# Index columns of gathers and scatters set by VectorE from PSUM tables, one packed schedule word for GpSimd, four splits placed after the second routing

## The chip, the cores and the metric

One NeuronCore of a Trainium2 chip runs the whole program. The metric is the device time of one launch in microseconds (us); the median of several runs is compared.

## The reference

The input is q, k and v (batch 4, 8 heads, 576 rows, head width 64). Attention runs within chunks of 64 rows; its output is a matrix x of 2304 tokens by 512. Two mixtures of 8 experts follow, each with top-1 routing, hidden width 1024 and a relu. The second keeps at most 576 tokens for each expert.

```python
def mixture(x, w_gate, w1, w2):              # twice; the first also scales by an output gate
    logits = x @ w_gate                      # 2304 x 8
    e = argmax(logits); gate = softmax(logits)[e]
    for each expert: out[rows of e] = gate * (relu(x[rows] @ w1[e]) @ w2[e])
```

Everything is float32, and so is the output (2304 x 512).

## The kernel before

The engines run separate programs that wait on semaphores. Four stages follow one another: attention with the first router's logits, the first routing, the expert tiles of mixture m=0, then the second routing and the expert tiles of mixture m=1.

**Routing (L701 to L792, VectorE).** It takes the argmax of the logits, ranks the tokens within their expert by matmuls, gives each expert whole tiles of 128 slots, and makes tables with one column for each tile (NTAB columns, 128 partitions): `gather_at` (the token row that each slot reads), `scatter_at` (the row that it writes), `gates`, `owner` (the tile's expert). Every instruction in `link(...)` is waited for before the next is issued. From `owner_f` it also works out a schedule for GpSimd (called POOL in the profile): `pieces[m][g]` and `pieces[m][g+1]` say from which to which weight piece GpSimd has to work in step g, and `middles[m][g]` where the scatter and the gather stand between them. The last instruction (L791) raises `routed`, for which TensorE's first transposes of gathered rows (L993), VectorE's `x_split` and GpSimd's third gather wait. `index_ready`, after L763, releases the first gather earlier.

**Weights.** A product is made of three matmuls (L998 to L1000) of a high and a low part, so that each weight piece (128 x 1024, 512 KB, 8 for each expert, 128 in all) goes through three steps: SyncE loads it into a ring of four slots, ScalarE copies it rounded into `wh` (L607; for an expert two further on, only when the last tile of the expert that holds the space has been multiplied), and GpSimd subtracts into `wl` (L423, called a split here). A split frees the ring slot. The pieces have one order through both mixtures. The first 12 are split during attention. In m=0 the schedule covers pieces 12 to 76. Pieces 76 to 80 (the second half of expert 1 of m=1) are split in the second routing, between its first and second gather (L497 to L499), and m=1's schedule starts at 80.

**A tile's way.** There are 20 tiles in each mixture. GpSimd gathers 128 rows into `xg` (indirect DMA, L514, or L488 for the first three). TensorE transposes them (L993), VectorE splits them into high and low parts (L812, L814), TensorE makes the first product (L998 to L1000), VectorE the relu (L804), TensorE transposes (L1020), VectorE splits (L821, L827), TensorE makes the second product, VectorE scales it into `y` (L842), and GpSimd scatters `y` (L528). In m=0 TensorE and VectorE also make the next router's logits of `y` (L1039, L835, L1045, L846), which the scatter writes along. TensorE's step g is: transposes of tile g, first product of tile g+1, transposes of the rows of tile g+2, second product of tile g. There is one `xg`, one `y`, one `gidx` and one `sidx`: L842 of tile j waits until the scatter of tile j-1 has landed (`y_out`), and the gather of tile g waits for the transposes of tile g-1 (`xT_done`).

**GpSimd's step g (L532 to L541)**, in program order: three loads of schedule values into registers (`due`, L434 to L436), the splits from lo to middle (at most 4), the scatter of tile g-1, the gather of tile g+3 (not in the last two steps), the splits from middle to hi. Before the scatter it copies a column of `scatter_at` into `sidx` (L522) and waits for its own copy, and before the gather a column of `gather_at` into `gidx` (L511), since the indirect DMA takes its indices from a fixed address.

Of the kernel before, what the change touches and what calls it, by code (L numbers as in the profile page):

```python
# [13 lines left out]
P = 128  # L14
# [9 lines left out]
def build(nc, q, k, v, wg1, wog1, w1a, w2a, wg2, w1b, w2b, cap, out):  # L24
# [31 lines left out]
    with ctx:  # L56
# [61 lines left out]
        scatter_at = [sb(f"scatter_at{m}", [P, NTAB], I32) for m in range(2)]  # L118
# [3 lines left out]
        pieces = [sb(f"pieces{m}", [P, NTAB], I32) for m in range(2)]  # L122

        middles = [sb(f"middles{m}", [P, NTAB], I32) for m in range(2)]
# [57 lines left out]
        ps_rank, ps_slot, ps_gate = b6, b7, b45  # L182

# [69 lines left out]
        si_here = [sem(f"si_here{m}") for m in range(2)]  # L253
# [141 lines left out]
        def _(pool):  # L395
# [35 lines left out]
            def due(m, g):  # L431


                lo = pool.value_load(at(pieces[m], g)[0:1, :], min_val=PX, max_val=2 * E * PX)  # L434
                hi = pool.value_load(at(pieces[m], g + 1)[0:1, :], min_val=PX, max_val=2 * E * PX)
                middle = pool.value_load(at(middles[m], g)[0:1, :], min_val=PX, max_val=2 * E * PX)  # L436
                return lo, middle, hi
# [14 lines left out]
            for m in range(2):  # L452
# [44 lines left out]
                if m == 1:  # L497
                    for i in range((E + 1) * PX + PW, (E + 2) * PX):
                        low_parts(i, i % RING)  # L499
                    pool.wait_ge(s_zero, 16 * NT)  # L500
# [5 lines left out]
                def gather(g):  # L506

                    if reached(g, 1):
                        pool.wait_ge(g_in[m], g * 16)
                        pool.wait_ge(xT_done[m], g)  # L510
                    nc.gpsimd.tensor_copy(gidx[:, :], at(gather_at[m], g)).then_inc(gi_here[m], 1)  # L511
                    pool.wait_ge(gi_here[m], g - 2)
                    stand_alone(pool)
                    nc.gpsimd.indirect_dma_start(xg[:, 0:src.shape[1]], None, src,  # L514
                                                 bass.IndirectOffsetOnAxis(ap=gidx[:, 0:1], axis=0),
                                                 bounds_check=N - 1, oob_is_err=False).then_inc(g_in[m], 16)

                def scatter(g):

                    if reached(g, 1):  # L520
                        pool.wait_ge(y_out[m], g * 16)
                    nc.gpsimd.tensor_copy(sidx[:, :], at(scatter_at[m], g)).then_inc(si_here[m], 1)  # L522
                    pool.wait_ge(si_here[m], g + 1)
# [111 lines left out]
        def _(dve):  # L635
# [65 lines left out]
            for m in range(2):  # L701
# [64 lines left out]
                for k in range(2):  # L766
# [16 lines left out]
                done = FIRST if m == 0 else (E + 2) * PX  # L783
                link(nc.vector.tensor_scalar_add(pace[:, 0:MT], pace[:, 0:MT], float(m * E * PX)))
                link(nc.vector.tensor_scalar(pieces[m][:, 1:MT + 1], pace[:, 0:MT], float(done), float(2 * E * PX),
                                             ALU.max, ALU.min))
                link(nc.vector.memset(pieces[m][:, 0:1], done))
                link(nc.vector.scalar_tensor_tensor(out=middles[m][:, 0:MT], in0=pieces[m][:, 0:MT], scalar=float(PW),
                                                    in1=pieces[m][:, 1:MT + 1], op0=ALU.add, op1=ALU.min))
                link(nc.vector.tensor_scalar(padding[:, :], slot_n[:, :], 0.0, float(SKIP), ALU.is_equal, ALU.mult))  # L790
                nc.vector.scalar_tensor_tensor(out=scatter_at[m][:, :], in0=padding[:, :], scalar=-1.0,  # L791
# [7 lines left out]
                def relu(j, half):  # L799
# [4 lines left out]
                    nc.vector.tensor_scalar_max(h[:, cols], ps_h[:, cols], 0.0).then_inc((h0_here, h1_here)[half][m], 1)  # L804

# [31 lines left out]
                def scaled(j):  # L837

                    dve.wait_ge(y_done[m], j + 1)
                    if reached(j, 1):  # L840
                        dve.wait_ge(y_out[m], j * 16)
                    nc.vector.tensor_scalar(y[:, 0:D], ps_y, at(gates[m], j), None, ALU.mult).then_inc(y_here[m], 1)  # L842
# [5 lines left out]
                def step(g, head=False, tail=False):  # L848
# [18 lines left out]
                    if not tail:  # L867
                        relu(g + 1, 1)
                        x_split(g + 2)
# [232 lines left out]
```

## Time and profile before

| | |
|---|---|
| three runs | 753.7, 753.04, 751.76 us (median 753.04) |
| the profiled execution | 754.11 us |
| its span in the trace | 752.4 us |
| TensorE busy | 642.0 us, 85% |
| VectorE busy | 356.8 us, 47% |
| ScalarE busy | 180.3 us, 24% |
| GpSimd busy | 419.8 us, 56% |
| TensorE's mean granted clock | 0.929 |

All times in the rows are from the start of the span. Attention ends near 108, the first tile of m=0 starts at 124, the second routing is from 433 to 459, and the rest is m=1. Busy shares are means over these stages. The splits alone (L423) are 302 us of GpSimd's time. A row of the timeline is: start, duration, engine, line, operation, output and inputs, and in brackets the engine's idle time before it with what ended it.

### The profile page before, as it was taken

How to read it: one execution, taken by the hardware profiler on the slowest of the kernel's cores; microseconds unless marked ns; L12 is line 12 of the kernel's file. 1: busy time of each engine (PE TensorE's matmuls, PEld its weight loads, DVE VectorE, ACT ScalarE, POOL GpSimd, SP SyncE). 2: the span in 40 equal slices, each digit the busy share in tenths (PEclk: the TensorE clock that was granted, in tenths of full speed). 3: DMA queues.
4: the chain of work that ended last, by engine and by line, in shares of the span. 5: the costliest groups of instructions: out<-in, count | busy, mean ns of one | idle time of the engine just before them, and what ended most of it. 6: DMA issues, size and time to landing. Idle time of an engine off the chain costs nothing.

```text
span 752.4 us, 15054 instructions
## 1 busy us (share of the span) xinstructions
PE 642.0 (85%) x4310; PEld 529.1 (70%) x4311; DVE 356.8 (47%) x652; ACT 180.3 (24%) x223; POOL 419.8 (56%) x351
## 2 busy tenths in 40 slices
PE   4898855999999999999987534999999999998653
PEld 3787844788887888877876423788888878886542
DVE  3887745454354354354334084545454364433240
ACT  2577631002420112422322200022023200243200
POOL 1046442256685657779778342116657763579760
PEclk9999985999999999999998655999999999999796
DMA  9999993043444425445554313114325532355500
GB/s 198 233 297 283 271 337 125 29 140 137 157 156 152 154 79 174 175 154 186 178 176 155 110 37 104 44 34 153 126 87 177 182 126 84 112 174 195 191 32 21
DMA packets 79690, 111.64 MB, mean 148 GB/s; under 512 B 28249, under 2 KB 46681, under 8 KB 79664
## 3 DMA queue, kind: packets, MB, share of 16 engines
q1 hardware_dynamic: 67616, 86.00, 37.0%
q0 software_dynamic: 8000, 25.17, 9.9%
q10 hardware_dynamic: 4048, 0.12, 0.3%
q8 instruction: 17, 0.28, 0.2%
q14 instruction: 9, 0.07, 0.0%
HBM read 92.48 MB, written 20.00 MB: 150 GB/s over the span
## 4 chain that ended last, share of the span: by engine, by line
PE 50%; POOL 14%; issue 12%; DVE 10%; POOLq 5%; DMA 5%; ACT 1%; ACTq 1%; DVEq 0%; SPq 0%
PE b L998 12%; PE b L999 12%; POOL wl L423 12%; PE b L1000 12%; PE b L925 2%; PE b L1020 2%; PE b L993 2%; PE b L903 2%; DVE owner L773 1%; DVE kT L665 1%; POOLq L423 1%; PE b L1045 1%; DVE xrow L676 1%; DMA x<-y,sidx 1%; PE b L913 1%
## 5 line engine op out<-in xcount | busy, mean ns | idle before, releaser
L423 POOL TENSOR_TENSOR wl<-ring,wh (+1 forms) x128 | 302.0, 2386 | 43.0 <-issue 21.3
L607 ACT CAST wh<-ring 128x1024 f32 (+1 forms) x112 | 112.8, 1047 | 479.2 <-PE b L1000 387.3
L998 PE MATMUL b<-wh,xTh 128*128 x320 | 135.0, 422 | 5.7 <-DVE xTl L814 3.7
L998 PE MATMUL b<-wh,hTh 128*128 x320 | 132.5, 414 | 7.5 <-DVE hTl L827 7.5
L842 DVE TENSOR_SCALAR y<-b,gates 128x512 f32<-128x512 f32 x40 | 30.0, 751 | 227.0 <-PE b L1000 103.2
L999 PE MATMUL b<-wh,xTl 128*128 x320 | 129.0, 403 | 0.0
L999 PE MATMUL b<-wh,hTl 128*128 x320 | 128.9, 403 | 0.0
L1000 PE MATMUL b<-wl,xTh 128*128 x320 | 128.0, 400 | 0.0
L1000 PE MATMUL b<-wl,hTh 128*128 x320 | 127.9, 400 | 0.0
L804 DVE TENSOR_SCALAR h<-b 128x512 f32<-128x512 f32 x80 | 54.8, 689 | 78.3 <-PE b L1000 78.1
L998 PEld LDWEIGHTS b<-wh,hTh 128*128 128x128 f32 x320 | 61.8, 193 | 21.3 <-issue 7.7
L998 PEld LDWEIGHTS b<-wh,xTh 128*128 128x128 f32 x320 | 61.6, 193 | 19.1 <-issue 7.2
L1000 PEld LDWEIGHTS b<-wl,hTh 128*128 128x128 f32 x320 | 61.3, 192 | 15.1
L1000 PEld LDWEIGHTS b<-wl,xTh 128*128 128x128 f32 x320 | 61.3, 192 | 14.8
L999 PEld LDWEIGHTS b<-wh,hTl 128*128 128x128 f32 x320 | 61.8, 193 | 12.8
L999 PEld LDWEIGHTS b<-wh,xTl 128*128 128x128 f32 x320 | 61.8, 193 | 11.4
L514 POOL DMA_INDIRECT xg<-x,gidx x36 | 37.8, 1049 | 31.4 <-POOL gidx L511 30.5
L827 DVE TENSOR_TENSOR hTl<-b,hTh 128x512 fp32r<-128x512 f32 x80 | 52.7, 680 | 0.0
L821 DVE CAST hTh<-b 128x512 fp32r<-128x512 f32 x80 | 51.1, 681 | 0.0
L993 PE MATMUL b<-ident,xg 128*128 128x128 f32 x168 | 26.8, 284 | 25.2 <-DMA xg<-x,gidx 12.2
L427 POOL DMA_DIRECT2D x<-xrow x18 | 10.2, 566 | 63.3 <-DVE xrow L676 63.3
L993 PEld LDWEIGHTS b<-ident,xg 128*128 128x128 f32 x168 | 21.5, 147 | 32.3 <-DMA xg<-x,gidx 13.5
(142 smaller groups left out, 663.1 us busy)
## 6 DMA issues: line engine op xcount, KB each, us to landing
ring<-in_moe_w SPq DMA_DIRECT2D x128, 512.0 KB, 3.2
vin<-in_v SPq DMA_DIRECT2D x72, 64.0 KB, 4.9
x<-xrow POOLq DMA_DIRECT2D x18, 256.0 KB, 6.1
out<-zeros SPq DMA_DIRECT2D x18, 256.0 KB, 3.8
qin<-in_q SPq DMA_DIRECT2D x6, 512.0 KB, 7.5
kin<-in_k SPq DMA_DIRECT2D x6, 512.0 KB, 6.9
qin<-in_q SPq DMA_DIRECT2D x2, 384.0 KB, 5.6
kin<-in_k SPq DMA_DIRECT2D x2, 384.0 KB, 5.9
```

What stands on the lines that cost most here:

```text
L423: nc.gpsimd.tensor_tensor(low, src, high.bitcast(F32), ALU.subtract).then_inc(wl_here, 1)
L514: nc.gpsimd.indirect_dma_start(xg[:, 0:src.shape[1]], None, src, bass.IndirectOffsetOnAxis(ap=gidx[:, 0:1], axis=0), bounds_check=N - 1, o ...
L607: nc.scalar.copy(dst, ring[:, i % RING]).then_inc(wh_here, 1)
L804: nc.vector.tensor_scalar_max(h[:, cols], ps_h[:, cols], 0.0).then_inc((h0_here, h1_here)[half][m], 1)
L821: nc.vector.tensor_copy(hTh[:, chunks, :], ps_hT[:, half * BANK:(half + 1) * BANK].rearrange("p (c t) -> p c t", t=P)).then_inc((hTh0_here ...
L827: nc.vector.tensor_tensor(hTl[:, chunks, :], ps_hT[:, half * BANK:(half + 1) * BANK].rearrange("p (c t) -> p c t", t=P), hTh[:, chunks, :] ...
L842: nc.vector.tensor_scalar(y[:, 0:D], ps_y, at(gates[m], j), None, ALU.mult).then_inc(y_here[m], 1)
L903: last = nc.tensor.transpose(ps_aT[:, c * P:(c + 1) * P], xrow[:, (t - 1) % XS, c].rearrange("p e d -> p (e d)"), ident[:, :])
L993: last = nc.tensor.transpose(ps_xT[:, c * P:(c + 1) * P], xg[:, c * P:(c + 1) * P], ident[:, :])
L998: nc.tensor.matmul(dst, high, weights(wh, *wt), start=start, stop=False)
L999: nc.tensor.matmul(dst, low, weights(wh, *wt), start=False, stop=False)
L1000: return nc.tensor.matmul(dst, high, weights(wl, *wt), start=False, stop=stop)
```

## The change

- `due` loads one word, `schedule[m][g]`, which is lo + 256 middle + 65536 hi, and takes it apart in registers. VectorE makes the word in the routing with two more linked instructions. `pieces` and `middles` become float tables that both mixtures share.
- VectorE writes the two index tables into PSUM (`ps_gather`, `ps_scatter`, both in the bank b7, behind the columns that the routing's matmuls use there): one more linked instruction for `ps_gather`, while `scatter_at` becomes `ps_scatter`. `gather_at` stays in SBUF for the first three gathers.
- The copies into `gidx` and `sidx` move from GpSimd to VectorE: `next_rows(g + 3)` in VectorE's step g, after the relu of tile g+1 and before `x_split(g + 2)`, and the `sidx` copy in `scaled(j)`, after its waits and before L842. GpSimd's waits on `g_in`, `xT_done`, `y_out` and `si_here` ahead of these copies go with them. It now waits for `gi_here`, raised by VectorE, and for `y_here`.
- The four splits L497 to L499 leave the second routing. m=1's schedule starts at piece 76, so they come in its steps.

```diff
--- before.py
+++ after.py
@@ -115,13 +115,13 @@
 
         gates = [sb(f"gates{m}", [P, NTAB]) for m in range(2)]
         gather_at = [sb(f"gather_at{m}", [P, NTAB], I32) for m in range(2)]
-        scatter_at = [sb(f"scatter_at{m}", [P, NTAB], I32) for m in range(2)]
         ends = [sb(f"ends{m}", [P, E + 1], I32) for m in range(2)]
         owner = [sb(f"owner{m}", [P, NTAB], I32) for m in range(2)]
 
-        pieces = [sb(f"pieces{m}", [P, NTAB], I32) for m in range(2)]
-
-        middles = [sb(f"middles{m}", [P, NTAB], I32) for m in range(2)]
+        pieces = sb("pieces", [P, NTAB])
+
+        middles = sb("middles", [P, NTAB])
+        schedule = [sb(f"schedule{m}", [P, NTAB], I32) for m in range(2)]
 
         ring = sb("ring", [P, RING, PIECE])
 
@@ -180,6 +180,7 @@
         ps_pT, ps_aT = b6, b7
         ps_h, ps_hT, ps_y, ps_yT, ps_xT = b01, b23, b45[:, 0:BANK], b45[:, BANK:2 * BANK], b6
         ps_rank, ps_slot, ps_gate = b6, b7, b45
+        ps_gather, ps_scatter = b7[:, 2 * P:2 * P + NTAB], b7[:, 3 * P:3 * P + NTAB]
 
         s_const = sem("s_const")
         s_tables = sem("s_tables")
@@ -250,7 +251,6 @@
         yT_here = sem("yT_here")
         yl_done = sem("yl_done")
         yl_here = sem("yl_here")
-        si_here = [sem(f"si_here{m}") for m in range(2)]
         y_out = [sem(f"y_out{m}") for m in range(2)]
 
         w1_dram = [w.rearrange("e (c p) f -> e p c f", p=P) for w in (w1a, w1b)]
@@ -431,9 +431,8 @@
             def due(m, g):
 
 
-                lo = pool.value_load(at(pieces[m], g)[0:1, :], min_val=PX, max_val=2 * E * PX)
-                hi = pool.value_load(at(pieces[m], g + 1)[0:1, :], min_val=PX, max_val=2 * E * PX)
-                middle = pool.value_load(at(middles[m], g)[0:1, :], min_val=PX, max_val=2 * E * PX)
+                cuts = pool.value_load(at(schedule[m], g)[0:1, :], min_val=0, max_val=2 ** 24 - 1)
+                lo, middle, hi = pool.snap(cuts % 256), pool.snap(cuts // 256 % 256), pool.snap(cuts // 65536)
                 return lo, middle, hi
 
             def split(lo, hi):
@@ -495,8 +494,6 @@
                 pool.wait_ge(index_ready, m + 1)
                 gather_first(0)
                 if m == 1:
-                    for i in range((E + 1) * PX + PW, (E + 2) * PX):
-                        low_parts(i, i % RING)
                     pool.wait_ge(s_zero, 16 * NT)
                 gather_first(1)
                 pool.wait_ge(routed, m + 1)
@@ -505,10 +502,6 @@
 
                 def gather(g):
 
-                    if reached(g, 1):
-                        pool.wait_ge(g_in[m], g * 16)
-                        pool.wait_ge(xT_done[m], g)
-                    nc.gpsimd.tensor_copy(gidx[:, :], at(gather_at[m], g)).then_inc(gi_here[m], 1)
                     pool.wait_ge(gi_here[m], g - 2)
                     stand_alone(pool)
                     nc.gpsimd.indirect_dma_start(xg[:, 0:src.shape[1]], None, src,
@@ -517,10 +510,6 @@
 
                 def scatter(g):
 
-                    if reached(g, 1):
-                        pool.wait_ge(y_out[m], g * 16)
-                    nc.gpsimd.tensor_copy(sidx[:, :], at(scatter_at[m], g)).then_inc(si_here[m], 1)
-                    pool.wait_ge(si_here[m], g + 1)
                     pool.wait_ge(y_here[m], g + 1)
                     if m == 0:
                         pool.wait_ge(yl_here, g + 1)
@@ -780,15 +769,20 @@
                 link(nc.vector.tensor_scalar(near[:, 0:MT], near[:, 0:MT], float(PW), float(PX + PW), ALU.mult, ALU.add))
                 link(nc.vector.scalar_tensor_tensor(out=pace[:, 0:MT], in0=owner_f[:, 0:MT], scalar=float(PX),
                                                     in1=near[:, 0:MT], op0=ALU.mult, op1=ALU.add))
-                done = FIRST if m == 0 else (E + 2) * PX
+                done = FIRST if m == 0 else (E + 1) * PX + PW
                 link(nc.vector.tensor_scalar_add(pace[:, 0:MT], pace[:, 0:MT], float(m * E * PX)))
-                link(nc.vector.tensor_scalar(pieces[m][:, 1:MT + 1], pace[:, 0:MT], float(done), float(2 * E * PX),
+                link(nc.vector.tensor_scalar(pieces[:, 1:MT + 1], pace[:, 0:MT], float(done), float(2 * E * PX),
                                              ALU.max, ALU.min))
-                link(nc.vector.memset(pieces[m][:, 0:1], done))
-                link(nc.vector.scalar_tensor_tensor(out=middles[m][:, 0:MT], in0=pieces[m][:, 0:MT], scalar=float(PW),
-                                                    in1=pieces[m][:, 1:MT + 1], op0=ALU.add, op1=ALU.min))
+                link(nc.vector.memset(pieces[:, 0:1], float(done)))
+                link(nc.vector.scalar_tensor_tensor(out=middles[:, 0:MT], in0=pieces[:, 0:MT], scalar=float(PW),
+                                                    in1=pieces[:, 1:MT + 1], op0=ALU.add, op1=ALU.min))
+                link(nc.vector.scalar_tensor_tensor(out=middles[:, 0:MT], in0=pieces[:, 1:MT + 1], scalar=256.0,
+                                                    in1=middles[:, 0:MT], op0=ALU.mult, op1=ALU.add))
+                link(nc.vector.scalar_tensor_tensor(out=schedule[m][:, 0:MT], in0=middles[:, 0:MT], scalar=256.0,
+                                                    in1=pieces[:, 0:MT], op0=ALU.mult, op1=ALU.add))
                 link(nc.vector.tensor_scalar(padding[:, :], slot_n[:, :], 0.0, float(SKIP), ALU.is_equal, ALU.mult))
-                nc.vector.scalar_tensor_tensor(out=scatter_at[m][:, :], in0=padding[:, :], scalar=-1.0,
+                link(nc.vector.tensor_scalar(ps_gather, slot_n[:, :], -1.0, 0.0, ALU.add, ALU.max))
+                nc.vector.scalar_tensor_tensor(out=ps_scatter, in0=padding[:, :], scalar=-1.0,
                                                in1=slot_n[:, :], op0=ALU.add, op1=ALU.add).then_inc(routed, 1)
 
                 def gates_copy():
@@ -802,6 +796,11 @@
                         dve.wait_ge((hT0_done, hT1_done)[half][m], j)
                     cols = slice(half * BANK, (half + 1) * BANK)
                     nc.vector.tensor_scalar_max(h[:, cols], ps_h[:, cols], 0.0).then_inc((h0_here, h1_here)[half][m], 1)
+
+                def next_rows(g):
+
+                    dve.wait_ge(xT_done[m], g)
+                    nc.vector.tensor_copy(gidx[:, :], at(ps_gather, g)).then_inc(gi_here[m], 1)
 
                 def x_split(j):
 
@@ -839,6 +838,7 @@
                     dve.wait_ge(y_done[m], j + 1)
                     if reached(j, 1):
                         dve.wait_ge(y_out[m], j * 16)
+                    nc.vector.tensor_copy(sidx[:, :], at(ps_scatter, j))
                     nc.vector.tensor_scalar(y[:, 0:D], ps_y, at(gates[m], j), None, ALU.mult).then_inc(y_here[m], 1)
 
                 def logits_copy(j):
@@ -866,6 +866,7 @@
                         logits_copy(g - 1)
                     if not tail:
                         relu(g + 1, 1)
+                        next_rows(g + 3)
                         x_split(g + 2)
                     scaled(g)
                     if m == 0 and tail:
```

## Rows read from the trace of the kernel before

**Rows 1.** Waits of all engines: waiter, waited for, us in total, times, longest

```profile
DVE y L842 <- DMA out<-y,sidx: 63.9, 7, 17.4
```

**Rows 2.** Timeline, second routing (start us, duration us, work)

```profile
445.69 10.02 DVE L773 TENSOR_SCALAR owner<-owner_f 128x28 int32<-128x28 f32 x1
446.42 9.24 POOL L423 TENSOR_TENSOR wl<-ring,wh 128x1024 fp32r<-128x1024 f32 x4
...
459.29 1.11 PE L993 MATMUL b<-ident,xg 128*128 128x128 f32 x4 [11.34 <-DVE scatter_at L791]
```

**Rows 3.** Timeline, first routing, the same three places

```profile
120.30 0.18 DVE L773 TENSOR_SCALAR owner<-owner_f 128x28 int32<-128x28 f32 x1
...
123.17 0.19 DVE L791 SCALAR_TENSOR_TENSOR scatter_at<-padding,slot_n 128x28 int32<-128x28 f32 x1
...
124.27 1.11 PE L993 MATMUL b<-ident,xg 128*128 128x128 f32 x4 [1.70 <-DMA xg<-x,gather_at]
```

**Rows 4.** Timeline of POOL alone, one step of m=0

```profile
330.27 0.18 POOL L522 COPY sidx<-scatter_at 128x1 int32 x1
331.38 1.02 POOL L528 DMA_INDIRECT x<-y,sidx  x1 [0.93 <-POOL sidx L522]
332.39 0.20 POOL L511 COPY gidx<-gather_at 128x1 int32 x1
333.46 1.05 POOL L514 DMA_INDIRECT xg<-x,gidx  x1 [0.86 <-POOL gidx L511]
336.10 9.46 POOL L423 TENSOR_TENSOR wl<-ring,wh  x4 [1.59 <-ACT wh L607]
```

**Rows 5.** Line 434, one of the three loads: ns min/median/max

```profile
L434 POOLq TENSOR_LOAD <-pieces x40: 285/295/420, 136.8 to 727.6; - x40
```

**Rows 6.** Chain of work from 202 to 206: start, us, what

```profile
202.93 0.53 issue
```

**Rows 7.** Timeline of PE, m=0: transposes L1020 of tiles 0, 12, 13, 19

```profile
136.03 1.17 PE L1020 MATMUL b<-ident,h 128*128 128x128 f32 x8
...
303.81 1.04 PE L1020 MATMUL b<-ident,h 128*128 128x128 f32 x8
...
317.65 1.03 PE L1020 MATMUL b<-ident,h 128*128 128x128 f32 x8
...
406.46 1.03 PE L1020 MATMUL b<-ident,h 128*128 128x128 f32 x8
```

**Rows 8.** Timeline of DVE, m=0: L842 of tiles 18 and 19

```profile
409.31 0.75 DVE L842 TENSOR_SCALAR y<-b,gates 128x512 f32<-128x512 f32 x1 [6.68 <-DMA x<-y,sidx]
...
422.88 0.75 DVE L842 TENSOR_SCALAR y<-b,gates 128x512 f32<-128x512 f32 x1 [8.29 <-PE b L1000]
```

**Rows 9.** Stretch in m=0's last product: us, busy times, then PEclk, DMA share, GB/s

```profile
416.00:418.00 2.00, 2.00 (x6) 1.52 (x5) 0.00 (x0) 0.00 (x0) 2.00 (x1) 0.50 0.69 195
```

**Rows 10.** Timeline of PE, m=1: gathered tiles 12 and 19, transposes of tiles 13, 14

```profile
605.54 0.66 PE L993 MATMUL b<-ident,xg 128*128 128x128 f32 x4 [1.66 <-DMA xg<-x,gidx]
...
636.68 1.03 PE L1020 MATMUL b<-ident,h 128*128 128x128 f32 x8
...
649.20 1.03 PE L1020 MATMUL b<-ident,h 128*128 128x128 f32 x8
...
702.77 1.11 PE L993 MATMUL b<-ident,xg 128*128 128x128 f32 x4 [9.40 <-DMA xg<-x,gidx]
```

**Rows 11.** Timeline of POOL, m=1: splits of steps 15 and 16, scatter of 17

```profile
663.50 9.48 POOL L423 TENSOR_TENSOR wl<-ring,wh  x4 [1.99 <-ACT wh L607]
...
677.25 18.82 POOL L423 TENSOR_TENSOR wl<-ring,wh  x8
...
727.68 1.03 POOL L528 DMA_INDIRECT out<-y,sidx  x1 [0.94 <-POOL sidx L522]
```

**Rows 12.** Timeline of DVE, m=1: L842 of the last tile

```profile
741.30 0.75 DVE L842 TENSOR_SCALAR y<-b,gates 128x512 f32<-128x512 f32 x1 [7.57 <-PE b L1000]
```

**Rows 13.** Line 846, a small copy from PSUM: ns min/median/max

```profile
L846 DVE COPY y<-b x20: 166/166/167, 156.3 to 426.2; 128x8 f32<-128x8 f32 x20
```

## The prediction

> **What bounds the kernel now.** I read the waits first, then the timeline in three places. Busy shares name no bound: TensorE is busy for 85% of the span and GpSimd for 56%, but each is late in other stretches. Among the waits, VectorE's L842 (y) stands waiting for landed scatters of m=1, 63.9 us in 7 waits [rows 1]. A scatter is late only when GpSimd comes late to it. So the questions are where GpSimd's step is longer than TensorE's, and what else holds the path.
>
> Second routing: L773, a 128x28 instruction, takes 10.02 us [rows 2]; the same instruction in the first routing takes 0.18 [rows 3]. It ends at 455.71, and the four splits of GpSimd beside it end at 455.66 [rows 2]. The first routing has no splits beside it. TensorE then waits for `routed` until 459.29 [rows 2], so all of it is on the path.
>
> m=0: TensorE's tile takes 13.84 us when nothing is late (303.81 to 317.65) [rows 7]. GpSimd's step with four splits takes 15.24: in rows 4 the copy 0.18 and its wait 0.93, the scatter 1.02, the copy 0.20 and its wait 0.86, the gather 1.05, a gap of 1.59, and four splits of 9.41 in all. GpSimd is the bound wherever such steps follow one another. From tile 12 to 19 TensorE needs 102.65 us [rows 7], where seven tiles of 13.84 are 96.9: 5.8 us lost. From tile 0 to 12 it needs 167.8 against 166.1: 1.7 lost [rows 7]. At the end y of tile 18 waits for a scatter until 409.31, and y of tile 19 comes at 422.88 [rows 8], 16.4 us after tile 19's transposes; TensorE makes that last product at the granted clock of 0.50 (1.2 of 2.4 GHz) [rows 9].
>
> m=1: TensorE's tile takes 12.52 [rows 10]. It is stopped once for 1.66 by a late gather and once for 9.40 [rows 10], and at the end y of tile 18 is late again behind the scatter of tile 17 at 727.68 [rows 11].
>
> **The change part by part.**
>
> *Splits out of the second routing.* Without them L773 should take the 0.18 of the first routing and end at 445.87. From its end to the end of L791 the first routing takes 123.36 - 120.48 = 2.88 [rows 3]. Three linked instructions are new (two to pack the word, one for `ps_gather`), each of about 0.22 with its link, as L773 to L791 go (13 links in 2.88): 0.66 in all. L791 ends at 449.4, and TensorE starts 0.7 later (459.29 against L791's end), at 450.1. The other bound is the gather: in the first routing TensorE starts on the landed gather 3.97 after L773's start [rows 3], which gives 449.7 here, so it is covered. Gain 459.29 - 450.1 = 9.2. In the first routing the same three instructions cost 0.66, of which the gather's landing, by which TensorE waits there [rows 3], hides a part; bounds 0 and 0.66, I take 0.4.
>
> The trace shows one VectorE instruction held through four splits [rows 2]. The Trainium skill ("SBUF — State Buffer", "Who interferes with whom") says that a `tensor_scalar` with both operands in SBUF can take the port pair that VectorE shares with GpSimd, and that the second to come fully blocks; by that rule the stall goes with the splits, as the rows say.
>
> *Where the four splits land.* m=1's schedule now gives pieces 76 to 80 to step 1, ahead of the scatter of tile 0 and the gather of tile 4. They cost 9.4 there [rows 4]. TensorE makes expert 0's first tiles then, the scatter has to land only by the next y, a tile (12.5) after the last, and the gather waits for TensorE's transposes anyway. The splits run from about 482 to 492 in old times, the scatter lands some 3 us later, and the next y comes at 497.5. Cost 0, with 2.5 us to spare. SyncE's loads for expert 2 come later by as much and still ahead of ScalarE's need. If that cover were gone, it would cost up to 9.4.
>
> *Copies moved off GpSimd.* Each step loses 1.11 (330.27 to 331.38) and 1.07 (332.39 to 333.46) [rows 4]. That counts the wait: 0.53 of it is the sequencer preparing the indirect DMA after the copy [rows 6], which can now run ahead under the splits, since its semaphores stand long before. Of the gap of 1.59, two loads go, each 0.29 [rows 5] with about 0.3 of register work behind it; the divisions add something that no row shows, a few register operations. Bounds for the gap: 0 (all hidden) and 1.6 (the divisions eat the gain); I take 0.65, so 0.95 less. A step with four splits comes to 15.24 - 2.18 - 0.95 = 12.1, below both 13.84 and 12.52.
>
> VectorE gains two copies of 128x1 out of PSUM in a step. The nearest row is L846, also out of PSUM, at 0.166 [rows 13]. The `gidx` copy waits for the same transposes as the split of x behind it; what is queued behind is x_split, which TensorE needs a second product (about 6 us) later. The `sidx` copy delays y by 0.19; behind it stand the splits of the hidden tile, with over 4 us to spare, and in m=0 the transposes L1039, with 0.9. Both hidden, except once at each mixture's end: 0.4 in all. The gather now waits for VectorE in place of TensorE, 0.2 to 0.3 later, for rows needed a tile later: 0.
>
> *What that gives in m=0.* With steps of 12.1 every scatter lands within 0.3 of the moment that y wants, which the 0.9 covers, so both losses go: 1.7 + 5.8 = 7.5. At the end TensorE no longer stands still for 2.7 us before tile 18's logits, and its clock should stay up. Then y of tile 19 follows the transposes by 11.1 (0.6 + 0.9 to y of tile 18, 3.6 to its logits' end, 5.6 to 6 for the product) instead of 16.4: gain 5.3. With the clock down, as now, it is 2.5. I take 5.
>
> *What it gives in m=1.* The wait of 1.66 [rows 10] goes, since the gather before it leaves 5 us earlier: 1.7 to 1.9, I take 1.9. Steps 15 to 18 start from a split at 663.50 that ScalarE and TensorE set [rows 11] and stay there. Four splits end at 672.9; scatter and gather end at 675.1 in place of 677.2; eight splits in a row [rows 11] end at 693.9; scatter 694.0, gather 695.0 in place of 699.3, landed at 698.4. TensorE waits for it 5.2 instead of 9.4 [rows 10], and the second product of tile 17 starts at 700.2 (hidden splits behind y at 697.3) instead of 703.9. Then four splits from 696.8 to 706.2, scatter, gather to 708.3, and splits of the last four pieces from 709.0 (ScalarE can round them only after tile 17's product at 706.9) to 718.4. The scatter of tile 17 goes at 718.45 instead of 727.68 [rows 11], lands at 721.5, and y of the last tile follows by the same path as now, so 741.30 [rows 12] becomes 732.3. Gain 9.0, with 2 more if the clock stays up in the last product.
>
> *Sum.* 9.2 - 0.4 + 7.5 + 5 + 1.9 + 9.0 - 0.4 = 31.8. The span of 752.4 becomes 720.6 and the profiled run of 754.11 becomes 722.3. The median of the runs is 1.07 below that run, so I predict 753.04 - 31.8 = 721.2.
>
> **The rivals.**
>
> *The DMA can't be prepared ahead.* The gap between copy and DMA might be the DMA's own and be paid after any instruction. For: each indirect DMA of rows 4 shows it, and a scatter that waits for y shows 0.9 too. Against: the 0.53 stands behind the copy's semaphore [rows 6], and GpSimd's sequencer reads on while splits run. The copies then save only 0.2 each and the step is 13.9 long. m=0 still gets 7.1 + 4, m=1's end only 3.0 (steps 15 to 18: seven copies of 0.2 and two gaps of 0.8). Sum 9.2 - 0.4 + 7.1 + 4 + 1.9 + 3.0 - 0.6 = 24.2: 728.8. The Trainium skill ("Advanced Engine Details and Errata", "Sequencer Loop") has engine instructions queued while the sequencer reads on, which would speak for my forecast; no row shows a DMA queued so.
>
> *The copies are held by splits (slower).* If a 128x1 copy with integer output is held through a run of splits as L773 was (9.84 longer) [rows 2, 3], y waits on VectorE until the run ends. There are 29 runs of four splits behind the routings. With 4 us to spare in m=1 and 0.9 in m=0, a y that falls at a run's start would cost 5 to 8 us, perhaps 12 times: some 75. Then 753 - 22 + 75 = 806. It decides from 31.8 / 29 = 1.1 us of TensorE's time for each run. Against: L842 and L846 read PSUM under splits and are never stretched (0.166 to 0.167) [rows 13]; for: neither writes integers.
>
> *The packed word doesn't pay.* If the divisions take 1 us, the gap stays 1.6 and the step is 13.1, still below 13.84 but above 12.52. Only m=1's end notices: 2 us less, 723.
>
> **How the numbers follow.** Forecast with its variants of gap and clock 0.77, the unprepared DMA 0.15, held copies 0.05, no net change through a cover I misjudged 0.03. The range: below, 2.2 for the last product's clock, 1 for gaps hidden and 1 for the run: 717. Above, the second case and 2 for spread: 731. A difference of over 0.3% is what a measurement of this kernel can tell from none: faster 0.93, same 0.02, slower 0.05.
>
> **What would show it.** L773 near 0.18 in both routings, and TensorE's first transposes of m=1 about 4.4 us after it. GpSimd's step with four splits at 12.1 wherever it isn't waiting, with the scatter 0.1 behind the last split (0.9 would be the first rival). TensorE 13.84 a tile through all of m=0, and one wait of some 5 us for a gather in m=1. `sidx` and `gidx` copies near 0.16; any of several us is the slower case. I am wrong if splits in step 1 delay the first tiles, or if VectorE's copies show up ahead of TensorE's waits.

## The result and the profile after

The changed kernel takes 732.89 us (median of 4 runs, 731.08 to 733.94) against 753.37 (4 runs), a ratio of 0.972 with a 95% interval of 0.969 to 0.976. Timed a second time on another occasion it took 730.84 us (ratio 0.966, 0.964 to 0.968). I had forecast 721.2, with 717 to 731 as the range. The sign and most of the mechanisms were right; the gain was 20 to 25 us instead of 32.

The stages, read off the timelines of two profiled executions of each kernel. A stage begins and ends at the start of the instruction named.

| stage, us | before | after | forecast gain | gain |
|---|---|---|---|---|
| start to GpSimd's first copy of the gates in the first routing | 117.45, 121.23 | 120.41, 118.22 | 0 | none clear |
| to the first transposes of rows, m=0 | 6.82, 6.83 | 7.47, 7.48 | -0.4 | -0.65 |
| to the hidden transposes of tile 0 | 11.76, 11.75 | 11.71, 11.39 | 0 | 0.2 |
| to those of tile 19 | 270.43, 270.56 | 265.84, 265.56 | 7.5 | 4.8 |
| to the last y of m=0 | 16.42, 16.20 | 14.93, 14.81 | 4.8 | 1.4 |
| to the same copy of the gates, second routing | 19.97, 19.99 | 20.04, 20.10 | 0 | -0.1 |
| to the first transposes of rows, m=1 | 16.44, 16.44 | 7.28, 7.28 | 9.2 | 9.2 |
| to the hidden transposes of tile 0 | 11.54, 11.64 | 10.64, 10.60 | 0 | 1.0 |
| to those of tile 17 | 215.91, 216.06 | 214.00, 214.01 | 1.9 | 2.0 |
| to those of tile 18 | 23.87, 23.76 | 23.53, 23.50 | 3.8 | 0.3 |
| to those of tile 19 | 14.31, 14.44 | 12.52, 12.51 | 1.4 | 1.9 |
| to the last y, m=1 | 16.38, 16.30 | 12.63, 12.63 | 3.6 | 3.7 |
| to the end | 11.10, 11.10 | 11.10, 11.11 | 0 | 0 |

The two profiled executions of before took 754.11 and 758.01 us. Three rows hold the shortfall: m=0's tiles, m=0's end, and tile 17 to 18 of m=1. One row gave 1.0 that I hadn't forecast.

The second routing after the change, from the timeline of all engines (it answers rows 2):

```profile
442.81 1.13 POOL L487 DMA_INDIRECT xg<-x,gather_at  x1 [1.19 <-DVE gather_at L752]
...
443.24 0.18 DVE L762 TENSOR_SCALAR owner<-owner_f 128x28 int32<-128x28 f32 x1
...
446.77 0.20 DVE L785 SCALAR_TENSOR_TENSOR b<-padding,slot_n 128x28 f32<-128x28 f32 x1
447.68 1.11 PE L994 MATMUL b<-ident,xg 128*128 128x128 f32 x4 [2.19 <-DVE b L785]
```

L762 is the old L773. It takes 0.18, and TensorE starts 4.44 after it, still released by VectorE and not by the gather, as the 4.4 of the forecast had it.

GpSimd's steps in m=0, from its own timeline (they answer rows 4):

```profile
347.08 1.02 POOL L517 DMA_INDIRECT x<-y,sidx  x1
348.41 1.03 POOL L507 DMA_INDIRECT xg<-x,gidx  x1 [0.30 <-issue]
349.46 9.42 POOL L423 TENSOR_TENSOR wl<-ring,wh  x4
359.04 1.02 POOL L517 DMA_INDIRECT x<-y,sidx  x1 [0.17 <-DVE gidx L803]
360.37 1.02 POOL L507 DMA_INDIRECT xg<-x,gidx  x1 [0.31 <-issue]
361.42 9.44 POOL L423 TENSOR_TENSOR wl<-ring,wh  x4
371.44 1.02 POOL L517 DMA_INDIRECT x<-y,sidx  x1 [0.59 <-issue]
```

From scatter to scatter it is 11.96 us. This first step isn't yet the one to compare with rows 4: its schedule is loaded under its splits, and the same step took 13.63 before (346.61 to 360.24). The next one is of the kind of rows 4, with the loads between the gather and the splits. It took 15.23 before (360.24 to 375.47). Now its last split ends 11.82 after its scatter starts, so that it takes 11.99 with the 0.17 that follow, and in the trace 12.40, since the next scatter starts 0.59 behind. The forecast was 12.1. The scatter starts 0.17 behind the last split where 1.11 lay between them [rows 4], and the gather 0.30 behind the scatter's end. So the sequencer does prepare an indirect DMA while splits run, and the first rival falls. By the Trainium skill ("Advanced Engine Details and Errata", "Sequencer Loop") engine instructions are queued while the sequencer reads on; the trace agrees.

VectorE's two new copies, by line (ns min/median/max):

```profile
L841 DVE CAST sidx<-b x40: 157/159/160, 153.6 to 720.9; 128x1 int32 x38, 128x1 int32<-128x1 f32 x2
L803 DVE CAST gidx<-b x38: 146/148/151, 148.1 to 703.1; 128x1 int32 x36, 128x1 int32<-128x1 f32 x2
```

None is held, though 32 of the 78 copies run beside splits, so the slower rival falls too. What was late instead shows in the waits of the whole execution. Before, rows 1 had 63.9 us in 7 waits for m=1, and for m=0 the same view had:

```profile
DVE y L842 <- DMA x<-y,sidx: 59.9, 10, 6.7
```

After:

```profile
DVE sidx L841 <- DMA out<-y,sidx: 47.2, 6, 16.3
...
DVE sidx L841 <- DMA x<-y,sidx: 23.1, 4, 6.1
```

VectorE still waits for landed scatters, 70.3 us instead of 123.8, although they leave earlier. In m=0, the first late one, and what TensorE (L1040) makes of it, from the timeline:

```profile
206.37 7.50 SPq L379 DMA_DIRECT2D ring<-in_moe_w  x3
206.37 1.02 POOL L517 DMA_INDIRECT x<-y,sidx  x1 [0.17 <-ACT wh L596]
...
211.07 0.16 DVE L841 CAST sidx<-b 128x1 int32 x1 [6.07 <-DMA x<-y,sidx]
211.20 0.75 DVE L842 TENSOR_SCALAR y<-b,gates 128x512 f32<-128x512 f32 x1
...
212.09 0.65 PE L1040 MATMUL b<-ident,y 128*128 128x128 f32 x4 [0.89 <-DVE y L842]
```

VectorE's copy, which waits for the landed scatter, starts 4.70 us after the scatter does. In before's 17 waits of this kind that took 2.9 to 3.4 us, of which the last 0.13 to 0.2 pass between landing and start. By landings it is 3.7 to 4.7 us here, in nine of ten waits, against 2.8 to 3.3. In the same hundredth of a microsecond SyncE issues a ring load (the first line), since the last split frees a ring slot and now nothing stands between it and the scatter. In before the load is issued 0.9 to 1.1 ahead of the scatter.

The same in m=1, around tile 19's gather:

```profile
680.15 1.02 POOL L517 DMA_INDIRECT out<-y,sidx  x1 [0.17 <-issue]
...
684.83 0.16 DVE L841 CAST sidx<-b 128x1 int32 x1 [16.27 <-DMA out<-y,sidx]
...
685.46 1.11 PE L994 MATMUL b<-ident,xg 128*128 128x128 f32 x4 [6.52 <-DMA xg<-x,gidx]
```

### The profile page after: what moved, and what is told of

Read it like the earlier page. It is cut to its first block, busy times and chain, and to the rows that moved or that the text cites. A ratio compares the mean times of both kernels' runs of the same rounds, so it can differ in the third digit from the quotient of the medians.

```text
span 732.1 us, 14755 instructions
## 1 busy us (share of the span) xinstructions
PE 643.7 (88%) x4310; PEld 532.4 (73%) x4311; DVE 356.3 (49%) x736; ACT 180.0 (25%) x223; POOL 406.3 (56%) x275
## 4 chain that ended last, share of the span: by engine, by line
PE 69%; DVE 10%; DMA 8%; issue 4%; POOL 3%; ACT 2%; POOLq 1%; ACTq 1%; DVEq 0%; SPq 0%
PE b L999 18%; PE b L1000 17%; PE b L1001 17%; PE b L1021 3%; DMA ring<-in_moe_w 3%; POOL wl L423 3%; DMA x<-y,sidx 3%; PE b L926 3%; PE b L994 2%; PE b L1046 2%; ACT wh L596 2%; PE b L904 2%; PE b L914 1%; DVE kT L654 1%; PE b L948 1%
## 5 line engine op out<-in xcount | busy, mean ns | idle before, releaser
L841 DVE CAST sidx<-b 128x1 int32 (+1 forms) x40 | 6.3, 159 | 201.5 <-PE b L1001 131.2
L517 POOL DMA_INDIRECT x<-y,sidx x20 | 20.4, 1020 | 48.9 <-DVE y L846 42.7
L517 POOL DMA_INDIRECT out<-y,sidx x20 | 20.3, 1013 | 45.5 <-DVE y L842 43.6
```

Source lines behind the costliest of these rows:

```text
L517: nc.gpsimd.indirect_dma_start(dst, bass.IndirectOffsetOnAxis(ap=sidx[:, 0:1], axis=0), y[:, 0:width], None, bounds_check=N - 1, oob_is_er ...
```

## The experiments: the parts of the change

Each part alone on the kernel before. I first asked whether the gains are where the forecast puts them.

**The splits alone.**

```diff
-                    for i in range((E + 1) * PX + PW, (E + 2) * PX):
-                        low_parts(i, i % RING)
...
-                done = FIRST if m == 0 else (E + 2) * PX
+                done = FIRST if m == 0 else (E + 1) * PX + PW
```

> The kernel before with one part of the change: the four splits leave the second routing and m=1's schedule starts at piece 76. If the 10.02 us of L773 were time held by splits and nothing else waits there, the second routing is shorter by 9.85 less nothing, since no linked instruction is added: 743.5 us against 753.4, L773 near 0.2. Rival, the splits only change place and come back in the first steps of m=1: 753.

744.95 us against 755.09, ratio 0.987 (0.982 to 0.992). The routing from the gates' copy to the first transposes of m=1 takes 6.59 instead of 16.44. The same instruction in the kernel with the splits out and in the one with only the columns moved (the next experiment), by VectorE's timelines:

```profile
443.30 0.18 DVE L771 TENSOR_SCALAR owner<-owner_f 128x28 int32<-128x28 f32 x1
```

```profile
440.67 10.01 DVE L766 TENSOR_SCALAR owner<-owner_f 128x28 int32<-128x28 f32 x1
```

So the hold comes with the splits and goes with them, and nothing comes back in m=1's first tiles (13.8 for the first and 12.51 for the next ones, as before). The 9.85 of this part is shown. How the hold begins is not: in rows 2 the held instruction starts 0.73 ahead of the first split's start, 0.42 behind the start of the gather, and in the kernel without the splits it takes 0.18 at the same distance from the gather. So the gather alone doesn't hold it, and by the profile the split had not started.

**The index columns alone.** The change's edits to the index tables, with before's three loads and its splits in the routing:

```diff
-                    nc.gpsimd.tensor_copy(gidx[:, :], at(gather_at[m], g)).then_inc(gi_here[m], 1)
...
-                    nc.gpsimd.tensor_copy(sidx[:, :], at(scatter_at[m], g)).then_inc(si_here[m], 1)
...
+                    nc.vector.tensor_copy(gidx[:, :], at(ps_gather, g)).then_inc(gi_here[m], 1)
...
+                    nc.vector.tensor_copy(sidx[:, :], at(ps_scatter, j))
```

> The kernel before with only the index columns moved to VectorE and PSUM. The schedule keeps its three loads, the routing its splits. If the parts add up, this one carries what is left of the 20.5 us after the splits' 9.9 and the word's share: GpSimd's step with four splits 13.1 instead of 15.24, and 742 us. If the later landing of the scatters (3.7 to 4.7 us in place of 3.0) comes with these columns, it shows here too. Rival, the gain of these stretches comes from the packed word: 750.

742.29 us, ratio 0.982 (0.977 to 0.987), as expected. m=0's tiles take 265.7 from tile 0 to 19, m=1's tile 17 to 18 takes 23.52 and the stretch to the last y 12.59, all as in the whole change. The late landings (3.8 to 4.7 us where VectorE waits for them) come with this part.

**The word alone,** with the instructions that pack it:

```diff
-                lo = pool.value_load(at(pieces[m], g)[0:1, :], min_val=PX, max_val=2 * E * PX)
-                hi = pool.value_load(at(pieces[m], g + 1)[0:1, :], min_val=PX, max_val=2 * E * PX)
-                middle = pool.value_load(at(middles[m], g)[0:1, :], min_val=PX, max_val=2 * E * PX)
+                cuts = pool.value_load(at(schedule[m], g)[0:1, :], min_val=0, max_val=2 ** 24 - 1)
+                lo, middle, hi = pool.snap(cuts % 256), pool.snap(cuts // 256 % 256), pool.snap(cuts // 65536)
```

> The kernel before with only the schedule packed in one word. The gap before the splits goes from 1.59 to about 0.7, the step from 15.24 to 14.4, still above TensorE's 13.84. m=0 gets back 3 us, m=1's end 1.5, the two routings cost 0.4 each for two more linked instructions: 749.5 us. Scatters land after 3.0 us, since the copy still stands between the last split and the scatter. Rival, the divisions cost what the loads saved: 754.

745.68 us, ratio 0.985 (0.980 to 0.990). I expected 749.5, so this missed by 4. The gap before the splits is the expected one, by GpSimd's timeline:

```profile
334.37 1.05 POOL L514 DMA_INDIRECT xg<-x,gidx  x1 [0.88 <-POOL gidx L511]
336.04 9.47 POOL L424 TENSOR_TENSOR wl<-ring,wh  x4 [0.62 <-ACT wh L607]
```

0.62 in place of 1.59, and landings in m=1 of 2.6 to 3.3 us. What I had sized wrongly is m=0: its tiles take 265.7 here too, and its end 14.53 instead of 16.4. A step of the kind of rows 4 takes 14.30 here (360.26 to 374.56), as expected, but the step ahead of it, with the load under the splits, takes 13.69 (346.57 to 360.26), and I had counted every step as the longer kind.

**Both but the word.** The parts alone give 10, 13 and 9 us, 32 in all; together they give 20 to 25. The changed kernel with the three loads back:

```diff
-                cuts = pool.value_load(at(schedule[m], g)[0:1, :], min_val=0, max_val=2 ** 24 - 1)
...
+                lo = pool.value_load(at(pieces[m], g)[0:1, :], min_val=PX, max_val=2 * E * PX)
```

> The changed kernel without the packed word: three loads as before, with the index columns on VectorE and the splits out of the routing. If the parts overlap because GpSimd's step without the copies is already shorter than TensorE's tile, the word adds nothing here: 733 us, as the changed kernel, while alone it gave 9. Rival, the parts add up (10, 13 and 9 us): 741.

733.49 us, ratio 0.972 (0.969 to 0.974). That is the ratio of the changed kernel's first timing, and 0.5% above that of its second. From GpSimd's first copy of the gates to the end the profile has 611.0 us, against 611.7 and 611.0 in the two of the changed kernel, so the difference isn't in the stages behind attention. The word is worth 9 us alone and nothing that the traces show on top of the columns: both shorten GpSimd's step, which takes 13.19 with three loads and no copies (356.21 to 369.40), and in m=0 what lies below TensorE's 13.85 brings nothing.

**The tables in SBUF.** The change puts them in PSUM. Is that why the copies aren't held?

```diff
-        ps_gather, ps_scatter = b7[:, 2 * P:2 * P + NTAB], b7[:, 3 * P:3 * P + NTAB]
+        ps_gather, ps_scatter = sb("table_g", [P, NTAB])[:, :], sb("table_s", [P, NTAB])[:, :]
```

> The changed kernel with its two index tables in SBUF instead of PSUM; VectorE still makes the 128x1 copies. If what held L773 (SBUF in and out, beside splits) holds these copies too, some of the 78 copies take up to 9.4 us, y and the rows of x come late, and the time is 750 to 800 us. Rival, a copy of one element for each partition isn't held, or only a wide one is: 732.9 us and copies near 0.15 us.

731.05 us, ratio 0.969 (0.963 to 0.974). The copies out of SBUF, by tile:

```profile
L841 DVE CAST sidx<-table_s x40: 153/154/155, 151.2 to 717.8; 128x1 int32 x38, 128x1 int32<-128x1 f32 x2
```

None of the 40 is held, nor any of the 38 into `gidx` (0.141 to 0.146); 32 of the 78 run beside splits. PSUM isn't needed here. The Trainium skill ("SBUF — State Buffer", "Who interferes with whom") lets `copy` and `tensor_scalar` take the shared port pair only when their operands meet the conditions of a two-port mode. The trace fits that: a 128x28 `tensor_scalar` was held and a copy of one column not. Whether the width decides wasn't tried.

## The experiments: why the scatters land late

Theory A: the scatter and the ring load start together, and the load's 512 KB keep the DMA engines busy. Theory B: the gather follows the scatter too closely (0.30 us instead of 1.06 with its copy). Both came with the same edit, so each is taken away by itself.

**Shorter ring loads.** Those of m=1 bring 128 of 1024 columns, so that m=1 multiplies with weights that mostly aren't there:

```diff
+                    if m == 1:
+                        dst, w = (dst[:, 0:P], w[:, 0:P]) if i < PW else (dst[:, 0:1, 0:P], w[:, 0:1, 0:P])
                     sp.dma_start(dst, w).then_inc(piece_in[i % RING], 16)
```

> The changed kernel with the ring loads of mixture 1 cut to 128 of 1024 columns (64 KB in place of 512 KB), so mixture 1 multiplies with wrong weights; its tiles are the same. Theory A: the scatters land after 3.7 to 4.7 us because they now start in the same moment as the ring load that the last split releases, and share the DMA engines with its 512 KB. Then the scatters of m=1 that stand right behind splits land after 2.8 to 3.1 us here, and tiles 17 to 18 take some 22 us instead of 23.5. Theory B: it is the gather, issued 0.3 us behind the scatter instead of 1.06; then the landings stay at 3.7 to 4.5.

The timeline around the scatter whose y is late before tile 19, as above:

```profile
677.79 1.01 POOL L519 DMA_INDIRECT out<-y,sidx  x1 [0.17 <-issue]
679.11 1.02 POOL L509 DMA_INDIRECT xg<-x,gidx  x1 [0.30 <-issue]
...
680.74 0.16 DVE L843 CAST sidx<-b 128x1 int32 x1 [14.51 <-DMA out<-y,sidx]
```

2.95 us from scatter to copy, where the changed kernel has 4.68, with the gather as close as there. Its profile gives landings of 2.6 to 2.8 for all scatters of m=1. The time is 729.63 us (one run). Tile 17 to 18 takes 21.61 instead of 23.5. The pieces for m=1 that are loaded at the end of m=0 are short as well, and m=0's end takes 12.42 instead of 14.9. Theory A.

**A filler ahead of the scatter,** an instruction of 0.82 us that nobody needs:

```diff
+                def fill(g):
+                    if reached(g, 1):
+                        pool.wait_ge(filled[m], g)
+                    nc.gpsimd.tensor_tensor(filler[:, 0:384], zeros[:, 0:384], zeros[:, 0:384], ALU.subtract).then_inc(filled[m], 1)
...
+                    fill(g)
                     if reached(g, 1):
                         scatter(g - 1)
```

> The changed kernel with a useless GpSimd instruction of about 0.9 us between the splits and the scatter, as far apart as the index copy had put them. Theory A: scatter and ring load are apart again, landing 3.0 us, so the landed row comes at about the same moment although the scatter goes 0.9 later. Theory B: landing stays at 3.7 to 4.5 and everything behind it comes 0.9 later; m=0 then loses another 1 to 2 us.

**The same filler ahead of the gather:**

```diff
+                        fill(g)
                         gather(g + 3)
```

> The changed kernel with the same filler of about 0.9 us between the scatter and the gather. Theory A: the scatter still starts with the ring load, landing 3.7 to 4.7 as in the changed kernel. Theory B: the gather is apart again and the scatter lands after 3.0 us; the waits of m=0 for a late y go away.

The landing of the same scatter in three kernels, by its line in a window of 1 us: with short loads, with the filler ahead of the scatter, with the filler ahead of the gather.

```profile
DMA to landing us min/median/max: 2.8/2.8/2.8
```

```profile
DMA to landing us min/median/max: 3.1/3.1/3.1
```

```profile
DMA to landing us min/median/max: 4.5/4.5/4.5
```

Moving the gather away changes nothing (733.44 us, one run); moving the scatter away from the load restores before's landing. The filler costs GpSimd 1 us in each step, and still the kernel took 730.24 us (one run), m=0's tiles 264.6 instead of 265.7 and tile 17 to 18 22.3 instead of 23.5. The last stretch shows the price: 14.1 instead of 12.6. Taken together, an instruction that does nothing is nearly free here: from the first copy of the gates to the end it is 610.6 us, against 611.7 and 611.0. The Trainium skill ("DMA: Bandwidth & Descriptors", "SWDGE vs HWDGE vs iDMA") says that transfers issued by GpSimd and by SyncE run on the same 16 DMA engines, which is how I read it. These runs show the size: the eleven scatters of m=1 that start with a load land 1.0 to 1.8 us later in the changed kernel's first profile than with short loads.

## The experiments: a better order

**y of m=1 later in VectorE's program.** A y that waits for a scatter also holds the split of the next tile's hidden values behind it.

```diff
                     hidden_low(g, 1)
+                    if m == 1 and reached(g, 1):
+                        scaled(g - 1)
...
-                    scaled(g)
+                    if m == 0 or tail:
+                        scaled(g)
```

(Step 1 is written out for m=1, so that every wait is for at least one scatter.)

> The changed kernel with y of m=1 made later in VectorE's program: behind the splits of the next tile's hidden values instead of ahead of them, so that a late scatter no longer holds them. If the wait for the landed scatter in front of y is what delays m=1's end, tile 17 to 18 takes 22.3 instead of 23.5 us, and from tile 19's transposes to the last y it takes 9 to 10 instead of 12.6: 4 us less in all, 729 against 732.9. Rival: the second product waits for y of the tile before as well, so only the order changes and the time stays at 733.

728.19 us, ratio 0.964 (0.962 to 0.966), the lowest of all kernels here, though its interval touches that of the changed kernel's second timing (0.964 to 0.968). In the trace tile 17 to 18 takes 21.21 (23.5) and the last stretch 12.00 (12.63), not the 9 to 10 that I expected. Why, from the timeline:

```profile
709.00 0.74 DVE L842 TENSOR_SCALAR y<-b,gates 128x512 f32<-128x512 f32 x1
710.03 0.79 PE L1011 MATMUL b<-wh,hTh 128*128 x1 [3.18 <-DVE y L842]
```

The last product waits for y of the tile before, which frees its bank, and then takes 7.41 us, to 717.44, where a product in a steady tile takes 5.84: TensorE had stood for 3.18, and from 710 to 717 its granted clock is 0.76.

**With the filler as well,** the line `fill(g)` ahead of the scatter added to the edit above.

> scaled_later (728.2 us) with the filler of 0.9 us ahead of the scatter, so that scatter and ring load are apart. If both findings add up, m=1's tile 17 to 18 takes 20.5 us instead of 21.2 and m=0's late tiles lose 1 us less: 726 to 727. Rival, the 0.9 us that the filler costs GpSimd in each step eats this: 728 to 729.

730.29 us, ratio 0.966 (0.964 to 0.969): tile 17 to 18 takes 21.8 and the last stretch 13.5. The two don't add up, as the rival said, and the time is above even its 728 to 729.

**Scatter and gather ahead of the splits.** `scalar=float(PW)` in the line of `middles` becomes `scalar=0.0`.

> The changed kernel with scatter and gather ahead of a step's splits (middles equal to lo). In m=1's end the scatter and gather of step 16 no longer stand behind its four splits, so that the gather of tile 19 leaves some 9 us earlier, in time for TensorE: tile 17 to 18 takes 12.5 to 16 us instead of 23.5. Then 722 to 725. Rival: in steps where GpSimd would wait for y the splits now wait as well, weights come late elsewhere, and it is 733 or more.

> The two together: scatter and gather ahead of the splits, and y of m=1 behind the hidden values. If a late scatter no longer happens at m=1's end, the second adds little: 720 to 724. If the last scatters are still late, it takes off 2 to 4 us more than scatter_first alone.

771.36 us, ratio 1.021 (1.016 to 1.025), and 772.46, ratio 1.021 (1.019 to 1.023). Slower than before: my expectation missed by 47 us, and its rival was right. The timeline of m=0, tile 4:

```profile
191.24 9.34 POOL L423 TENSOR_TENSOR wl<-ring,wh  x4
...
200.99 0.79 PE L999 MATMUL b<-wh,xTh 128*128 x1 [5.56 <-POOL wl L423]
...
209.16 1.02 POOL L517 DMA_INDIRECT x<-y,sidx  x1 [8.58 <-issue]
```

The splits that ran ahead of the scatter now run behind it, TensorE waits 5.56 us for weights, and GpSimd then stands idle for 8.58. Five times a tile takes about 21 us instead of 14. Tile 17 to 18 fell to 16.4 as hoped, and tile 18 to 19 rose to 25.4. The place of `middles` four splits in is what feeds TensorE.

**The two kernels once more,** for the first row of the table.

> The changed kernel itself, profiled once more. If the later end of attention (120.4 us in its first profile against 117.5) is spread between executions, it ends anywhere from 116 to 121 here and the rest of the stages repeats within 1 us. Rival, it belongs to the change: 120 to 121 again while before_again gives 117 to 118.

> The kernel before itself, profiled once more. Spread between executions: attention ends between 116 and 121. If it belongs to the change: 117 to 118.

The table's first row is 118.2 in the changed kernel and 121.2 in before, the other way round than in the first pair. In all 16 profiles, whose attention is the same, it lies between 116.4 and 121.2. It is spread between executions. The other stages of the two kernels repeat within 0.4 us.

## Why the prediction was off, step by step

- **Splits out of the routing.** Right: 9.2 forecast, 9.16 measured, and shown by the part alone. The three linked instructions cost 0.65 in the first routing, not 0.4: TensorE is now released by VectorE there, the gather hides nothing. The cover for the moved splits held.
- **Copies off GpSimd.** Right in the mechanism: the scatter 0.17 behind the splits, the step 12.0 to 12.5 (12.1), VectorE's copies 0.16 and hidden. The gap that the loads leave, forecast at 0.65, is 0.62 with the word alone. In the changed kernel it is 0.03 ahead of 361.42, where the load already ran beside the scatter (at 360.02), and 0.52 in a step at 221.19. That it can vanish is not in the forecast.
- **What that gives.** Here the step failed in which I let every scatter land 3 us after its issue "within 0.3 of the moment that y wants". I took the landing of before and moved it to a place where another transfer starts in the same moment. With 3.7 to 4.7 us instead of 3.0, y is late by more than the 0.9 of cover at three tiles of m=0, which lose 1.1, 1.2 and 0.5. The whole shortfall of these tiles, 2.7, is that. Their scatters landed after 4.6, 4.7 and 4.0; with 3.1 each y would come sooner by more than its tile lost, which is worked out and wasn't run. The filler, although it delays each scatter, gives back 1.1 of it.
- **m=0's end.** 1.4 instead of 4.8. TensorE stands for 1.67 twice, for y of tile 18 and for its copy behind the transposes, and its granted clock is at 0.50 (1.2 of 2.4 GHz) in the first part of the product, as in before. In the changed kernel, the stretch as in rows 9 but 4 us long:

```profile
410.00:414.00 4.00, 3.55 (x12) 3.20 (x13) 1.16 (x3) 0.00 (x0) 3.80 (x3) 0.50 0.69 250
414.00:418.00 4.00, 4.00 (x14) 3.15 (x13) 0.00 (x0) 0.00 (x0) 0.43 (x1) 0.69 0.58 200
```

I had assumed a clock that mostly stays up. With short loads the first of the two waits is gone and the stretch takes 12.42, 2.5 less. But the landing can't be given all of that. The two kernels with the scatter ahead of the splits have the same program in m=0 and y of tile 18 equally early, and take 14.01 and 12.42. With the filler ahead of the scatter, the scatter that tile 18 waits for lands after 2.9, and the stretch still takes 14.81, its last product at a mean granted clock of 0.66. So landing and clock together make the 3.4 that are missing, and the share of each stays open.

- **m=1's end.** 5.9 instead of 8.8 from tile 17 on, all of the difference in tile 17 to 18. 1.9 is the landing (short loads). The rest is for the most part the clock in the second product of tile 17, here its first matmul and the transposes behind its last:

```profile
687.84 0.79 PE L999 MATMUL b<-wh,hTh 128*128 x1 [1.26 <-DVE hTl L826]
...
695.85 1.03 PE L1021 MATMUL b<-ident,h 128*128 128x128 f32 x8
```

It took 8.0 us where I had put 6.7. It takes 7.9 with short loads too (mean granted clock 0.70), and 6.7 with the filler ahead of the scatter (0.83). The 6.7 was also counted from the wrong moment: before's product starts at 703.54 and not at 703.9, and takes 7.07. What follows tile 18 came as worked out.

- **The base.** I had three runs with a median of 753.04; later series of before gave medians of 755.1 to 756.2. Against those the gain is 25 us, and some 2 us of the miss in the time belong to the base. The stages behind attention, which don't hang on it, gave 23.7 of the 31.8.

The range ended at 731 and the first timing was 732.9. It held the case that a DMA can't be prepared ahead, which was false, and not the case that moving a DMA changes how long it takes.

What stays open: the first tile of m=1 came 1.0 us sooner in both profiles of the changed kernel; the same stretch is between 10.5 and 11.7 in the others, so I put it down to no cause.

## What to carry to other kernels

A DMA's time to landing is measured beside what ran next to it. When a change moves its issue, look at what the instruction in front of it releases: if that is another engine's load, the two now start together, and cover of under a microsecond is gone. Add the gains of parts that shorten the same engine only down to the point where the next engine is the bound, and try a do-nothing gap before moving work about.

## What the runs showed of the hardware

- One 128x28 VectorE instruction, SBUF to SBUF, was held for all four GpSimd instructions in a row beside it (10.0 us instead of 0.18), in each of the four profiles whose kernel keeps those splits. Copies of one column, out of PSUM or SBUF, were never held (0.141 to 0.164 us), though 31 to 39 of the 78 in each kernel ran beside splits.
- An indirect DMA behind other GpSimd work starts 0.17 us after it if its semaphores stand already. Behind a copy that it waits for, it starts 0.93 after that copy.
- What a scatter of 128 rows takes from issue to landing, in the profiles that record it and with loads of full size: 2.6 to 2.9 us in m=1 with no load issued within 4 us of it (up to 3.7 in m=0), 2.7 to 4.7 (median 3.1 to 3.2) with one issued 0.7 to 1.1 us ahead, 3.3 to 5.2 (median 3.6) with one 0.2 to 0.7 ahead, and 3.7 to 6.0 (median 4.3) when both are issued within 0.15 us.
